# Listing the busiest expert's first four slots inside the states' layer

## The chip, the cores and the metric

The kernel runs on one core of a Trainium2 chip. The metric is the device time of one execution in microseconds (us); lower is better. The engines are TensorE (PE in the profile, with its weight loads as PEld), VectorE (DVE), ScalarE (ACT), GpSimd (POOL) and SyncE (SP), which here only issues DMAs.

## The reference, cut to what matters

Three stages stand one after another. First an attention of 8 x 8 heads, 512 rows of x and 32 states each, in both directions; it gives 8 x (512 + 32) = 4352 rows of 512 numbers. Then a gated layer, then experts:

```
x   = concat(xread, sread)            # 8 batches x 544 rows, 512 wide
x   = ((x @ w_a) * (x @ w_b)) @ w_out # 512 -> 1536 -> 512
idx = argmax(x @ w_gate, axis=1)      # one of 8 experts for each row
for e in range(8):                    # w1[e]: 512 x 1024, w2[e]: 1024 x 512
    out[idx == e] = gate * (relu(x[idx == e] @ w1[e]) @ w2[e])
```

On these inputs the reference sends 1082, 32, 576, 64, 512, 1024, 512 and 550 rows to experts 0 to 7. Of the 4096 rows that come from x (the first 512 of each batch), expert 0 gets 1024 and expert 5 gets 1024; no other has more than 512.

## The kernel before, in words

**The gated layers.** Batches 0 to 7 go through attention and the gated layer with 512 columns each. A ninth pass, b = B, is the states' layer: the 256 state rows of all batches together. Each pass has 12 steps f. In a step TensorE makes a column block of x @ w_a into AB (`first_layer`, L1279), one of x @ w_b into BB, and adds the product of the step before to YB (`second_layer`, L1292). Between them stand fills of the bank pair FB, whose order is written out by hand in tables (`TURNS`, `HEADS`, ...): in the states' layer these turn the last batch's result ("yt") and make its logits ("lg"), four of each, in steps 0 to 3. VectorE forms the product in BB (L950) and its low half gl (L958); ScalarE copies AB (L711) and the high half gh (L719). TensorE needs gl of step f for its BB matmuls of step f + 1. All matrices are split in a rounded high part and a low part, so each product takes three matmuls.

**The routing.** After each step of the states' layer VectorE runs a piece of `route_early(f)`: the 32 tiles of 128 x-rows (T1 = 32 of T = 34 tiles) are ranked within their experts, from step 3 to step 11. TensorE counts with a triangular matrix in step 5 (L1346). After the layer come the two tiles of state rows: result to SBUF (L671), transposes (L1355), logits (L1363), counts (L1371), and a chain of small VectorE instructions (L1099 to L1158), in which every one waits for the one before. It gives each row a slot (one of SLOTS = 41 tiles of 128 rows, each of one expert) and a place in it. `match` and `carry` (L1121, L1129) and a GpSimd product (L562) make the table `what`; 34 matmuls `pick` x `what` (L1379) turn it into lists: `itab` (which rows of y to gather, where to scatter), `gates`, `etab` (the expert of a slot) and `ends` (the last slot of each expert).

**The experts' loop.** Slot j takes: GpSimd copies a column of `itab` to `cur` (L542), gathers 128 rows of y from DRAM into xg (L549), TensorE turns them (`turn_x`, L1392), `up` makes HB (24 matmuls, L1406), ScalarE applies relu (L771), `turn_h` turns it (L1428), `down` makes OB (24 matmuls, L1419), ScalarE scales (`result`, L782), GpSimd scatters (L555). TensorE's order in the loop is up(j), turn_x(j+1), down(j-1), turn_h(j). xg, xgh, hth and o_sb have one buffer each.

**The weights.** SP loads an expert's 8 MB in 16 chunks of 512 KB, in the order of the experts, into one of the two halves of WS (L474); at most two chunks are in flight, since chunk n waits for chunk n - 2. The first half of the chunks serves `up`, the second `down`. Expert 0 waits for the end of the last BB matmuls, and SP stores the last result rows before it (L344). From the third expert on, its load waits until the expert two before it has gone through its last `up` (first chunk) and `down` (ninth chunk):

```
end = eng.value_load(ends[0:1, e - 2:e - 1], min_val=0, max_val=SLOTS)
if e >= 2 and c == 0:
    eng.wait_ge(s["h_mm"], end * HALVES + 1)
if e >= 2 and c == CHUNKS // 2:
    eng.wait_ge(s["o_mm"], end + 1)
```

GpSimd's loop scatters the slot that lies LAG = 4 behind the one it gathers, right after the gather is issued, and ScalarE's result(j) waits for the scatter of slot j - 1.

Of the kernel before, what the change touches and what calls it, by code (L numbers as in the profile page):

```python
# [4 lines left out]
F32 = mybir.dt.float32  # L5
# [10 lines left out]
def attention_gated_experts(nc, x, state, w_a, w_b, w_out, w_gate, w1, w2, out):  # L16
# [29 lines left out]
    EARLY = 24  # L46
    LAG = 4
    MIDDLE = TOK // 2
# [21 lines left out]
    with ctx:  # L70
# [6 lines left out]
        def sem(name):  # L77
# [23 lines left out]
        closing = ExitStack()  # L101
        turned_end = sb("turned_end", [P, DM], F32, closing)
        closing.close()
# [7 lines left out]
        stage.close()  # L111
        wraw = sb("wraw", [P, 4, 512], F32, first)
# [25 lines left out]
        pick = sb("pick", [P, EARLY, P], F32R, early)  # L138
        e3 = {n: sb(n, [P, T, E], F32, early) for n in ("lt0", "lt1", "lt2")}
        one = sb("one", [P, T, E], BF16, early)  # L140
        tot = sb("tot", [P, E, T], F32, early)
        upto = sb("upto", [P, E, T], F32, early)
        tri = sb("tri", [P, 2, P], BF16, early)
        steps = sb("steps", [P, P], F32, early)
        rev = sb("rev", [P, E], F32, early)
        zeros = sb("zeros", [P, E * T], F32, early)
        tok = sb("tok", [P, T], F32, early)
        pt = sb("pt", [P, 8, T], F32, early)
        pe8 = sb("pe8", [P, 8, E], F32, early)
        pti = sb("pti", [P, 3, T], I32, early)  # L150
# [10 lines left out]
        listing = ExitStack()  # L161
        what = sb("what", [P, T, 3 * LIST], F32R, listing)
        late = sb("late", [P, T - EARLY, P], F32R, listing)
        same = sb("same", [P, T, LIST], F32, listing)
        gate2 = sb("gate2", [P, 2, T], F32R, listing)
        cmp41 = sb("cmp41", [P, SLOTS, E], F32, listing)
        f41 = sb("f41", [P, 5, SLOTS], F32, listing)
        itab = sb("itab", [P, SLOTS + LAG, 2], I32, listing)
        ends = sb("ends", [P, E], I32, listing)
        etab = sb("etab", [P, SLOTS], I32, listing)  # L170
        cur = sb("cur", [P, 2], I32, listing)
        gates = sb("gates", [P, SLOTS], F32, listing)
        listing.close()

        xg = sb("xg", [P, DM], F32, second)
        xgh, xgl = (sb(n, [P, KC, P], F32R, second) for n in ("xgh", "xgl"))
        h_sb = sb("h_sb", [P, FE], F32, second)
        hth, htl = (sb(n, [P, FEC, P], F32R, second) for n in ("hth", "htl"))
        o_sb = sb("o_sb", [P, DM], F32, second)
        HB = ps("HB", [P, HALVES, 512], second)  # L180
        HT = ps("HT", [P, 2, 512], second)
# [14 lines left out]
            "gp_turned", "iota_ready", "memory_free", "same_ready", "rows_ready", "early_mm", "early_read", "route", "shifted", "route_exp", "one_ready",  # L196
            "pick_ready", "what_ready", "list_mm", "list_ready", "taken",
# [3 lines left out]
        reads_out, reads_in = sem("reads_out"), sem("reads_in")  # L201
# [15 lines left out]
                 (10, 0): ("a2t", 1), (10, 3): ("sr", 1), (11, 1): ("a1t", 0), (11, 2): ("a1t", 1)}  # L217
        BEGIN = {(0, 0): ("a2t", 0), (0, 2): ("sr", 0), (1, 0): ("a2t", 1), (1, 2): ("sr", 1)}
# [25 lines left out]
        def table_of(b):  # L244
            t = {}
            if b == 0:
                t |= {k: (*v, 0) for k, v in BEGIN.items()}
            else:
                t |= {k: (*v, b - 1) for k, v in TURNS.items()}
# [129 lines left out]
        def _(eng):  # L379
# [44 lines left out]
            for b in range(NB):  # L424
                for f in range(FC):
                    if f == 0 and b % 2 and b < B - 1:
                        load_state(b // 2 + 1)
                    if f == 0 and b < B - 1:
                        load_x(eng, b + 1, 0)
# [12 lines left out]
            store_y(eng, B, 0)  # L442
            store_y(eng, B, 1)

            for e in range(E):
                for i in range(DEEP):
                    eng.wait_ge(piece_out[i], 16 * pieces_before(PIECES * (e + 1), i))
                if e == 0:  # L450
                    eng.wait_ge(s["b_done"], FC * NB)
                if e == 1:
                    eng.wait_ge(s["y_mm"], FC * NB)
                if e == 2:
                    eng.wait_ge(s["list_ready"], 1)
                if e >= 2:
                    end = eng.value_load(ends[0:1, e - 2:e - 1], min_val=0, max_val=SLOTS)
                for c in range(CHUNKS):
                    if e >= 2 and c == 0:
                        eng.wait_ge(s["h_mm"], end * HALVES + 1)  # L460
                    if e >= 2 and c == CHUNKS // 2:
                        eng.wait_ge(s["o_mm"], end + 1)
                    n = CHUNKS * e + c
                    if n >= 2:
                        eng.wait_ge(chunk_in[c % 2], 16 * (n // 2))
                    part, k = c // (CHUNKS // 4), c % (CHUNKS // 4)
                    dst = WS[:, e % 2, part * PART + k * CHUNK:part * PART + k * CHUNK + CHUNK].bitcast(F32)
                    if part == 0:
                        src = w1[e, k * P:k * P + P, :]
                    elif part == 2:  # L470
                        src, dst = w2_v[e, :, 2 * k:2 * k + 2, :], dst.rearrange("p (f d) -> p f d", f=2)
                    else:
                        src = lows[e, :, part // 2, k * CHUNK:k * CHUNK + CHUNK]
# [4 lines left out]
        def _(eng):  # L478
# [53 lines left out]
            eng.wait_ge(s["y_mm"], FC * NB)  # L532
            eng.wait_ge(s["y_evac"], T)
            for i in range(2):
                eng.wait_ge(y_stored[i], 16 * (B * TS // 2) + 16 * (P // N))
            for i in range(DEEP):
                eng.wait_ge(piece_out[i], 16 * pieces_before(PIECES * E, i))
            eng.memset(itab[:, :, :], 0).then_inc(s["memory_free"], 1)

            def take(k, n):  # L540

                eng.tensor_copy(cur[:, :], itab[:, bass.ds(k, 1), :].rearrange("p a b -> p (a b)"))\  # L542
                   .then_inc(s["taken"], 1)
                if whole(n):
                    eng.wait_ge(s["memory_free"], 1)
                eng.wait_ge(s["taken"], n)
# [5 lines left out]

            def scatter():

                eng.indirect_dma_start(out=out, out_offset=bass.IndirectOffsetOnAxis(ap=cur[:, 1:2], axis=0),  # L555
                                       in_=o_sb[:, :], in_offset=None, bounds_check=TOK - 1, oob_is_err=False)\
# [8 lines left out]

            eng.wait_ge(s["list_ready"], 1)
            for k in range(LAG):
                if k:
                    eng.wait_ge(s["turn_x"], k)
                take(k, k + 1)  # L570
                gather()
                eng.wait_ge(s["gathered"], 16 * k + 16)
            eng.wait_ge(s["list_ready"], 3)
            with eng.Fori(LAG + 1, SLOTS + 1) as n:
                eng.wait_ge(s["turn_x"], n - 1)
                eng.wait_ge(s["o_ready"], n - LAG)
                take(n - 1, n)
                gather()
                scatter()
                eng.wait_ge(s["gathered"], n * 16)  # L580
                eng.wait_ge(s["scattered"], n * 16 - 16 * LAG)
            for k in range(SLOTS, SLOTS + LAG):
                eng.wait_ge(s["o_ready"], k - LAG + 1)
                take(k, k + 1)
# [893 lines left out]
```

## Time and profile before

| | us |
|---|---|
| median of 3 runs (lowest, highest) | 1397.8 (1395.91, 1399.06) |
| the profiled execution | 1394.39 |
| its span, first to last instruction | 1392.7 |
| TensorE busy | 1323.2 (95%) |
| VectorE, ScalarE, GpSimd busy | 601.9, 509.1, 357.9 |
| states' layer, from its first AB matmul to its last YB matmul | 767.3 to 824.3 |
| first `up` matmul | 858.8 |

The span is that of one profiled execution; the 1.7 us between it and the execution's own time lie around the first and the last instruction. A busy TensorE is not one at its peak: the granted clock tells at which speed it ran. The chain that ended last says which engine's work set the end at each moment; idle time of the others costs nothing.

### The profile page before, as it was taken

What the parts mean: (1) busy time and instruction counts of PE and PEld (TensorE: products, weight loads), DVE (VectorE), ACT (ScalarE), POOL (GpSimd) and SP (SyncE); (2) the same over time, 40 slices, a digit from 0 to 9 for tenths busy, and PEclk for the clock granted to TensorE, in tenths of its full rate; (3) what the DMA queues carried; (4) which work ended last, traced back from release to release, by engine and by line L of the source; (5) the groups of instructions that cost most, each with busy time, mean ns of one, the idle gap of its engine ahead of it and who ended that gap; (6) DMA issues with size and microseconds to landing.
All of it is one profiled execution on the core that took longest, in us unless ns stands there. A gap on an engine that the chain in (4) does not pass through costs nothing.

```text
span 1392.7 us, 20352 instructions
## 1 busy us (share of the span) xinstructions
PE 1323.2 (95%) x6682; PEld 1099.3 (79%) x6683; DVE 601.9 (43%) x1070; ACT 509.1 (37%) x880; POOL 357.9 (26%) x350
## 2 busy tenths in 40 slices
PE   5899999999999999999999975999899999999996
PEld 3678888888888888778888974888787888888884
DVE  4775476664765755766556454111111111111110
ACT  4453354543545534546334210222122222222221
POOL 0001244443444523434233101111111111111111
PEclk9999999999999999999999986999999999999998
DMA  6231455445545554555467217713778772361100
GB/s 200 61 93 56 135 179 176 150 161 164 152 152 182 151 176 127 165 165 147 129 221 255 70 60 247 252 33 130 245 238 262 253 252 91 113 219 45 44 26 1
DMA packets 129085, 208.22 MB, mean 150 GB/s; under 512 B 47680, under 2 KB 49728, under 8 KB 129024
## 3 DMA queue, kind: packets, MB, share of 16 engines
q1 hardware_dynamic: 86336, 148.16, 33.3%
q10 hardware_dynamic: 36128, 39.59, 9.5%
q0 software_dynamic: 6560, 19.67, 4.4%
q8 instruction: 36, 0.59, 0.2%
q14 instruction: 25, 0.20, 0.0%
HBM read 155.47 MB, written 53.74 MB: 150 GB/s over the span
## 4 chain that ended last, share of the span: by engine, by line
PE 82%; DMA 8%; DVE 5%; issue 1%; SPq 1%; ACT 1%; POOL 0%; ACTq 0%; DVEq 0%; POOLq 0%
PE YB L1292 18%; PE OB L1419 14%; PE HB L1406 14%; PE BB L1279 10%; PE AB L1279 10%; DMA WS<-in_moe_w 5%; DMA WS<-expert_lows 3%; PE FB L1254 3%; DVE SW L814 2%; PE HT L1428 2%; PE FB L1205 2%; PE FB L1240 2%; PE FB L1225 2%; PE FB L1234 1%; PE XB L1392 1%
## 5 line engine op out<-in xcount | busy, mean ns | idle before, releaser
L510 POOL TENSOR_TENSOR raw<-raw,upper 128x512 f32<-128x512 f32 x128 | 167.7, 1310 | 254.7 <-DVE upper L832 254.7
L1406 PE MATMUL HB<-WS,xgh 128*128 x656 | 210.6, 403 | 8.6 <-DMA WS<-in_moe_w 6.8
L1419 PE MATMUL OB<-WS,hth 128*128 x656 | 206.5, 396 | 3.7 <-DVE htl L1168 2.8
L1168 DVE TENSOR_TENSOR htl<-HT,hth 128x1024 fp32r<-128x1024 f32 x41 | 50.2, 1225 | 301.9 <-ACT hth L775 301.9
L1292 PE MATMUL YB<-WOh,gh 128*128 128x512 f32 x408 | 165.3, 405 | 0.1
L1279 PE MATMUL AB<-ATh,SW 128*128 128x512 f32 (+1 forms) x480 | 160.5, 383 | 2.7 <-DVE ATl L906 2.7
L1279 PE MATMUL BB<-ATh,SW 128*128 128x512 f32 (+1 forms) x480 | 158.9, 380 | 2.2 <-DVE gl L958 1.5
L1292 PE MATMUL YB<-WOh,gl 128*128 128x512 f32 x408 | 159.8, 392 | 0.0
L1292 PE MATMUL YB<-WOl,gh 128*128 128x512 f32 x408 | 159.3, 390 | 0.0
L515 POOL TENSOR_TENSOR split_ring<-wr,split_ring 128x512 fp32r<-128x512 f32 x72 | 93.1, 1293 | 252.5 <-ACT split_ring L636 252.5
L1406 PEld LDWEIGHTS HB<-WS,xgh 128*128 128x128 f32 x656 | 123.0, 193 | 34.7 <-issue 9.7
L814 DVE TENSOR_TENSOR SW<-FB,SW 64x512 fp32r<-64x512 f32 x176 | 121.1, 688 | 51.4 <-ACT SW L629 47.7
L1419 PEld LDWEIGHTS OB<-WS,hth 128*128 128x128 f32 x656 | 120.3, 188 | 28.6 <-issue 5.0
L629 ACT ACTIVATE SW<-FB 64x512 fp32r<-64x512 f32 x176 | 104.2, 592 | 83.4 <-PE FB L1254 62.3
L1406 PE MATMUL HB<-WS,xgl 128*128 x328 | 130.7, 398 | 0.0
L1419 PE MATMUL OB<-WS,htl 128*128 x328 | 128.4, 391 | 0.0
L782 ACT ACTIVATE o_sb<-OB,gates 128x512 f32<-128x512 f32 x41 | 28.2, 689 | 265.9 <-DMA out_rows<-o_sb,cur 223.3
L542 POOL COPY cur<-itab 128x2 int32 (+1 forms) x45 | 8.4, 186 | 406.1 <-PE XB L1392 369.5
L950 DVE TENSOR_TENSOR BB<-gp,BB 128x512 f32<-128x512 f32 (+1 forms) x108 | 71.6, 663 | 77.9 <-PE BB L1279 77.0
L1279 PEld LDWEIGHTS AB<-ATh,SW 128*128 128x128 f32 x480 | 87.9, 188 | 19.5 <-DVE ATl L906 3.5
L1279 PEld LDWEIGHTS BB<-ATh,SW 128*128 128x128 f32 x480 | 88.0, 189 | 18.0 <-DVE gl L958 3.0
L719 ACT ACTIVATE gh<-BB 128x512 fp32r<-128x512 f32 (+1 forms) x108 | 61.8, 573 | 102.7 <-DVE BB L950 102.0
(179 smaller groups left out, 2054.2 us busy)
## 6 DMA issues: line engine op xcount, KB each, us to landing
raw<-in_moe_w SPq DMA_DIRECT2D x128, 256.0 KB, 3.1
expert_lows<-raw SPq DMA_DIRECT2D x128, 256.0 KB, 2.1
WS<-in_moe_w SPq DMA_DIRECT2D x64, 512.0 KB, 4.3
WS<-expert_lows SPq DMA_DIRECT2D x64, 512.0 KB, 4.6
wr<-in_moe_w_b ACTq DMA_DIRECT2D x52, 256.0 KB, 2.9
wr<-in_moe_w_a ACTq DMA_DIRECT2D x49, 256.0 KB, 3.1
y_rows<-y_sb ACTq DMA_DIRECT2D x32, 256.0 KB, 3.0
xq<-in_x SPq DMA_DIRECT2D x32, 128.0 KB, 3.2
```

What stands on the lines that cost most here:

```text
L510: eng.tensor_tensor(piece, piece, upper[:, :].bitcast(F32), ALU.subtract).then_inc(s["e_lo"], 1)
L515: eng.tensor_tensor(lower(a), src, rounded(a).bitcast(F32), ALU.subtract).then_inc(s["wf_lo"], 1)
L629: eng.activation(SW[r, j, side, m, :, 2 * (k // 2), :], bank[r, :].rearrange("p (f c) -> p f c", c=P), ACT.Copy).then_inc(s["sw_hi"], 1)
L719: eng.activation(gh[:, f % 2, 0:width], BB[:, 0:width], ACT.Copy)\
L814: eng.tensor_tensor(place[:, :, c + 1, :], bank[r, :].rearrange("p (f c) -> p f c", c=P), place[:, :, c, :].bitcast(F32), ALU.subtract).th ...
L950: eng.tensor_tensor(BB[:, 0:width], gp[:, 0:width], BB[:, 0:width], ALU.mult)\
L1168: eng.tensor_tensor(htl[:, :, :], HT[:, :, :].rearrange("p a (k c) -> p (a k) c", c=P), hth[:, :, :].bitcast(F32), ALU.subtract).then_inc( ...
L1254: last = eng.matmul(bank, part[:, k, :], w, start=(i == 0), stop=(i == 2))
L1279: last = eng.matmul(bank[:, 0:width], wt, act, start=(k == 0 and i == 0), stop=(k == len(terms) - 1 and i == 2))
L1292: last = eng.matmul(YB[:, tt, :], act[:, f % 2, c], wt[:, f, :], start=(f == 0 and i == 0), stop=(f == FC - 1 and i == 2))
L1406: last = eng.matmul(HB[:, i, :], act[:, k, :], w, start=(k == 0 and m == 0), stop=(k == KC - 1 and m == 2))
L1419: last = eng.matmul(OB[:, :], act[:, k, :], w, start=(k == 0 and m == 0), stop=(k == FEC - 1 and m == 2))
```

## The change

The 32 tiles of x-rows are counted earlier: the eight fills "yt" and "lg" of the last batch are packed into steps 0 to 2 (`TURNS_LAST`), and `route_early` runs from step 2. In step 5 `first_expert` picks the expert that most x-rows chose (the lowest index of equals) and writes `order`: this expert first, then the others in their order. Slots 0 to 3 (LAG = 4) then hold this expert's first 512 x-rows, whatever the state rows do. They are listed in step 9 by 32 small matmuls of 12 columns, and their gathers and matmuls no longer wait for the last ranking.

SP loads weights in the order of `order`, whose entry is read from SBUF into a register, so the DRAM address of each chunk comes from a register. The load of the first expert waits for `order_ready` and for the BB matmuls of step 3 (its first half) and step 7 (its second half), and no longer for the stores of the last rows. Those stores move to ScalarE's queue, behind the fourth gather; so that y holds something in those rows before, the states are copied there by one DMA (`spans`) when batch 7 begins.

After the layer TensorE's order is written out by hand: turn_x(0) ahead of the last `second_layer`, then up, down and turns of slots 0 to 3, and between them the transposes, logits, counts and the 34 list matmuls. VectorE's chain has the same steps as before and some 11 small ones more; `picks` makes 8 tiles in one instruction where it took one for each. In GpSimd's loop a scatter now lies BACK = 3 slots behind its gather, waits for `result` of its slot in the same turn, and the next turn's `take` waits for that scatter to land.

```diff
+        TURNS_LAST = {(0, 0): ("yt", 0), (0, 1): ("lg", 0), (0, 2): ("yt", 1), (1, 0): ("lg", 1),
+                      (1, 1): ("yt", 2), (1, 2): ("lg", 2), (1, 3): ("yt", 3), (2, 0): ("lg", 3)}
...
+                    if k == 0 and c % (CHUNKS // 2) == 0:
+                        eng.wait_ge(s["b_done"], B * FC + (4 if c == 0 else 8))
...
+                    one_of = bass.ds(e, 1)
                     if part == 0:
-                        src = w1[e, k * P:k * P + P, :]
+                        src = w1[one_of, i * P:i * P + P, :].rearrange("e p c -> (e p) c")
...
+            for k in range(LAG):
+                if k:
+                    eng.wait_ge(s["turn_x"], k)
+                take(k, k + 1 - BACK if k >= BACK else None)
+                gather()
+                eng.wait_ge(s["gathered"], 16 * k + 16)
+            eng.wait_ge(s["o_ready"], 1)
+            scatter()
             for i, (a, c) in enumerate(((0, T // 2), (T // 2, T))):
                 eng.wait_ge(s["same_ready"], i + 1)
                 eng.tensor_tensor(what[:, a:c, 0:LIST], ...)
...
+            with eng.Fori(LAG + 1 - BACK, SLOTS + 1 - BACK) as m:
+                eng.wait_ge(s["turn_x"], m + (BACK - 1))
+                eng.wait_ge(s["scattered"], m * 16 - 16)
+                take(m + (BACK - 1), m)
                 gather()
+                eng.wait_ge(s["memory_free"], 2)
+                eng.wait_ge(s["o_ready"], m)
                 scatter()
+                eng.wait_ge(s["gathered"], m * 16 + 16 * BACK)
...
+                if f == 7:
+                    picks(pick[:, 0:8, :], 0, 8)
...                    # gate, same_early, what_early: 10 small instructions
+                if f == 8:
+                    for a in range(8, T1, 8):
+                        picks(pick[:, a:a + 8, :], a, a + 8)
...
+                    if b == B and f == 9:
+                        eng.wait_ge(s["early_what"], 3)
+                        eng.wait_ge(s["early_read"], 1)
+                        for t in range(T1):
+                            if t % 8 == 0:
+                                eng.wait_ge(s["pick_ready"], t // 8 + 1)
+                            last = eng.matmul(RB[:, 0, 0:3 * LAG], pick[:, t, :], what_early[:, t, :],
+                                              start=(t == 0), stop=(t == T1 - 1))
+                        last.then_inc(s["early_list"], 1)
+                if b == B:
+                    eng.wait_ge(s["glo_ready"], FC * NB)
+                    turn_x(0)
                 second_layer(b, FC - 1, tiles)
...
+            up(0, 0, at, (0,))
             for tt in range(TN): ...          # transposes of the state tiles
+            turn_x(1)
+            up(0, 0, at, (1,))
             for tt ...                        # logits of the state tiles
+            turn_h(0)
+            up(1, 0, at, (0,))
...                                            # counts of the state tiles
+            up(1, 0, at, (1,))
+            turn_x(2)
+            down(0, 0, at)
+            turn_h(1)
+            up(2, 0, at)
+            turn_x(3)
             for t in range(T): ...            # the 34 list matmuls
+            down(1, 0, at)
+            turn_h(2)
+            up(3, 0, at)
+            turn_x(LAG)
+            down(2, 0, at)
+            turn_h(3)
```

## Rows read from the trace of the kernel before

**Rows 1.** The page: TensorE's granted clock in 40 slices of the span, tenths.
```profile
PEclk9999999999999999999999986999999999999998
```

**Rows 2.** Stretches: length, busy PE, PEld, DVE, ACT, POOL; granted clock, DMA share, GB/s.
```profile
824.30:858.70 34.40, 12.77 (x65) 11.62 (x64) 20.06 (x65) 2.50 (x5) 5.39 (x7) 0.56 0.72 223
...
845.00:849.00 4.00, 3.90 (x18) 3.70 (x17) 1.38 (x5) 0.00 (x0) 0.00 (x0) 0.50 0.76 248
...
1062.60:1067.00 4.40, 4.36 (x13) 3.42 (x14) 1.23 (x1) 1.22 (x2) 0.00 (x0) 0.64 0.81 253
```

**Rows 3.** The chain that ended last, in order of time: start, us, what.
```profile
822.66 1.67 PE YB L1292 x6
...
868.44 5.75 PE HB L1406 x24
874.19 0.44 PE XB L1392 x4
...
887.00 5.50 PE OB L1419 x24
892.50 0.87 PE HT L1428 x8
...
906.02 5.49 PE HB L1406 x24
...
983.41 8.19 PE HB L1406 x24
```

**Rows 4.** Timeline of GpSimd and TensorE around the first gather: start, us, instruction.
```profile
850.14 1.18 POOL L549 DMA_INDIRECT xg<-y_rows,cur  x1 [0.29 <-POOL cur L542]
...
855.91 1.09 PE L1392 MATMUL XB<-ident,xg 128*128 128x128 f32 x4 [6.85 <-DMA xg<-y_rows,cur]
```

**Rows 5.** Timeline of TensorE: logits of one tile; weight loads of ten list matmuls.
```profile
785.85 0.95 PE L1240 MATMUL FB<-wg,xt 128*128 128x8 f32 x8
...
846.62 2.25 PEld L1379 LDWEIGHTS RB<-what,late 128*128 128x128 f32 x10
```

**Rows 6.** VectorE's timeline: step 8 of the states' layer, and a 714-element comparison.
```profile
808.55 0.43 DVE L950 TENSOR_TENSOR BB<-gp,BB 128x256 f32<-128x256 f32 x1 [2.21 <-PE BB L1279]
809.43 0.42 DVE L958 TENSOR_TENSOR gl<-BB,gh 128x256 fp32r<-128x256 f32 x1 [0.45 <-ACT gh L719]
...
841.05 0.90 DVE L1121 TENSOR_TENSOR same<-steps,pt 128x714 f32<-128x714 f32 x1
```

**Rows 7.** The late ranking on VectorE, first, held and last instruction; GpSimd's product beside it.
```profile
831.50 0.16 DVE L1099 TENSOR_TENSOR pe<-pe,RB 128x8 f32<-128x8 f32 x1 [0.40 <-PE RB L1371]
...
837.36 1.38 DVE L1018 TENSOR_SCALAR pt<-pt 128x2 f32<-128x2 f32 x1
...
843.42 1.70 DVE L1129 TENSOR_TENSOR what<-same,gate 128x714 fp32r<-128x714 f32 x2
...
837.33 1.39 POOL L562 TENSOR_TENSOR what<-same,tok 128x714 fp32r<-128x714 f32 x1 [6.99 <-DVE same L1121]
```

**Rows 8.** SP's queue: the last rows' stores, first chunks of experts 0 and 1.
```profile
824.98 3.63 SPq L344 DMA_DIRECT2D y_rows<-y_sb  x8
828.78 5.74 SPq L474 DMA_DIRECT2D WS<-in_moe_w  x4
...
864.65 4.66 SPq L474 DMA_DIRECT2D WS<-in_moe_w  x3
```

**Rows 9.** Who TensorE waited for from 906 to 1370: us in total, times, longest.
```profile
PE HB L1406 <- DMA WS<-in_moe_w: 6.4, 2, 3.6
```

**Rows 10.** GpSimd, ScalarE and TensorE around one late scatter in the loop.
```profile
1108.48 1.00 POOL L549 DMA_INDIRECT xg<-y_rows,cur  x1 [0.75 <-POOL cur L542]
1109.79 1.01 POOL L555 DMA_INDIRECT out_rows<-o_sb,cur  x1 [0.31 <-issue]
...
1117.00 0.69 ACT L782 ACTIVATE o_sb<-OB,gates 128x512 f32<-128x512 f32 x1 [9.01 <-DMA out_rows<-o_sb,cur]
...
1120.32 0.73 PE L1419 MATMUL OB<-WS,hth 128*128 x2 [0.33 <-DMA WS<-in_moe_w]
```

More of the change, by code:

```diff
@@ L1281, in first_layer, with expert, turn_x @@
                 last.then_inc(s[done], 1)
+            def expert(j):
+                return eng.value_load(etab[0:1, bass.ds(j, 1)], min_val=0, max_val=E - 1)
+            def turn_x(j):
+                eng.wait_ge(s["gathered"], j * 16 + 16)
+                if not (isinstance(j, int) and j == 0):
+                    eng.wait_ge(s["xgl_ready"], j)
+                for k in range(KC):
+                    last = eng.transpose(XB[:, k * P:k * P + P], xg[:, k * P:k * P + P], ident[:, :])
+                last.then_inc(s["turn_x"], 1)
@@ new lines, in down @@
+            def down(j, e, at):
+                for c in chunk_in:
+                    eng.wait_ge(c, e * (8 * CHUNKS) + 8 * CHUNKS)
+                eng.wait_ge(s["htl_ready"], j + 1)
+                if not (isinstance(j, int) and j == 0):
+                    eng.wait_ge(s["o_ready"], j)
+                for k in range(FEC):
+                    for m, (act, half) in enumerate(((hth, 0), (hth, 1), (htl, 0))):
+                        w = WSf[:, bass.ds(at + ((2 + half) * PART + k * DM), DM)]
+                        last = eng.matmul(OB[:, :], act[:, k, :], w,
+                                          start=(k == 0 and m == 0), stop=(k == FEC - 1 and m == 2))
+                last.then_inc(s["o_mm"], 1)
@@ new lines, in turn_h, with slot_of @@
+            def turn_h(j):
+                eng.wait_ge(s["h_ready"], j * HALVES + HALVES)
+                if not (isinstance(j, int) and j == 0):
+                    eng.wait_ge(s["htl_ready"], j)
+                for k in range(FEC):
+                    last = eng.transpose(HT[:, k // 4, (k % 4) * P:(k % 4) * P + P], h_sb[:, k * P:k * P + P],
+                                         ident[:, :])
+                last.then_inc(s["turn_h"], 1)
+            def slot_of(e):
+                return eng.snap((e & 1) * (4 * PART))
@@ L1410, in down @@
-            def down(j, e, at):
-                for c in chunk_in:
-                    eng.wait_ge(c, e * (8 * CHUNKS) + 8 * CHUNKS)
-                eng.wait_ge(s["htl_ready"], j + 1)
-                if not (isinstance(j, int) and j == 0):
-                    eng.wait_ge(s["o_ready"], j)
-                for k in range(FEC):
-                    for m, (act, half) in enumerate(((hth, 0), (hth, 1), (htl, 0))):
-                        w = WSf[:, bass.ds(at + ((2 + half) * PART + k * DM), DM)]
-                        last = eng.matmul(OB[:, :], act[:, k, :], w,
-                                          start=(k == 0 and m == 0), stop=(k == FEC - 1 and m == 2))
-                last.then_inc(s["o_mm"], 1)
```

494 lines of the change are left out of this document (268 added, 226 removed).

## The prediction, on record before the change was run

> **What bounds the kernel now.** I read the page first: TensorE's granted clock is full nearly throughout and dips where the states' layer hands over to the experts [rows 1]. The table of stretches shows why: of the 34.4 us between the last YB matmul of the layer and the first `up`, TensorE works 12.8, at a mean clock of 0.56 [rows 2]. Then the chain that ended last, in order of time: up to 824.33 it is TensorE's layer, from 868.44 on TensorE's slots one after another [rows 3], and between the two SP's stores and the chunks of expert 0, from 824.98 on [rows 8]. So the ranking and the weights both fill the gap; removing one alone would leave the other. A slot of the steady loop is 5.49 (up) + 0.44 (turn_x) + 5.50 (down) + 0.87 (turn_h) = 12.30 us, without a pause [rows 3]. After slot 4 TensorE waits for weights only twice, 6.4 us in all [rows 9]. TensorE's order of work sets the end, so I count its timeline from the layer to the start of up(4), before and after.
>
> **Which expert comes first.** By the counts experts 0 and 5 tie with 1024 x-rows; the lowest index wins, and `order` is the order of before. Slots, loads and their collisions after slot 4 are therefore those of before, moved as a block: each later load starts from an `up` or `down` of TensorE.
>
> **Before, layer's end to up(4):** 906.02 - 824.33 = 81.7 us [rows 3].
>
> **After, the same work on TensorE, at full clock.** Four ups 22.0, three downs 16.5, four turn_h 3.5, turn_x of slots 1 to 4 1.8 [rows 3]; two groups of state transposes 0.9 (eight at 0.11, as in turn_x); 16 logit matmuls at 0.1, 1.6 [rows 5]; two counts 0.2; 34 list matmuls. These ran at a clock of 0.50 [rows 2] with a pitch of 2.25 / 10 = 0.22 us [rows 5]; at full clock I take half, so 3.7. Sum 50.2. What stands between: turn_x(1) needs a gather that starts when turn_x(0) is done. From issue at 850.14 to TensorE's start at 855.91 the first gather took 5.8, and some 0.7 goes before for the copy [rows 4]; behind turn_x(0) TensorE has the last YB group 1.7 [rows 3], half an up 2.75 and the transposes 0.9, 5.3 in all. Stall 1.2. Together 51.4.
>
> **The other engines beside it.** VectorE's late chain ran from 831.50 to 845.1, 13.6 us, of which some 2.4 went into two instructions held beside GpSimd's two products (one of them in [rows 7]). Without the holding, and with six added ranking steps of 0.2, two xl (1.4) and one hl (1.2), it is 15.0. From the counts to the list matmuls TensorE has half an up, turn_x, down, turn_h, up and turn_x: 2.75 + 0.44 + 5.5 + 0.87 + 5.5 + 0.44 = 15.5. The second half of `what` is wanted only after 17 of the list matmuls, at 17.4. So the ranking is hidden, by 2.4 us; uncovered, each us of it is a us of the sum. The tables behind it (1.3) and the fifth gather with its wait for the stores (6.5) lie under down(1), turn_h(2) and up(3), 11.9. GpSimd reaches its products after scatter 0, some 8 us behind turn_x(2), and needs 2.8 [rows 7] of a cover of 12.3. ScalarE's eight stores take 3.6 as SP's did [rows 8], while down(1) runs; queued behind them is result(1), not wanted for 5 us.
>
> **Weights.** `order` is ready after step 5, near 798.5 (step 8's low half is done at 809.85 [rows 6], three steps of 4.3 back is 797.0, then eight small instructions). 16 chunks took 864.65 - 828.78 = 35.9 [rows 8]: half by 817, all by about 836. up(0) starts near 828, down(0) near 844: hidden with 11 and 8 us to spare.
>
> **The longer layer.** 32 matmuls of 12 columns cost their weight loads, 0.10 to 0.11 at full clock [rows 5]: 3.5. turn_x(0) 0.4. "lg" 2 now waits for VectorE's copy of "yt" 2, about 0.3. In a step VectorE's product and low half are done 1.3 us after BB [rows 6], and TensorE wants the low half 2.8 after it, so 2.9 us of routing fit and 4.3 with the slack used up. Steps 2, 5 and 6 get 2.6 each, step 7 3.9 (a comparison of 1024 elements is 1.25 by the row of 714 in 0.90 [rows 6], and ten small ones), step 8 3 x 1.25 = 3.8. Steps 7 and 8 use the slack one after the other; the 0.3 too much falls under the early list. Layer +4.2; bounds 3.5 and 7.
>
> First gain: 81.7 - 51.4 - 4.2 = 26.1 us.
>
> **Corrections.** (a) Clock. After TensorE's first wait for weights an up took 8.19 in place of 5.49, 2.7 more [rows 3]; after the second the clock was 0.64 over 4.4 us, 1.6 more [rows 2]. The list matmuls of before, 7.7 us of them, never raised the clock from 0.50 [rows 2], so narrow ones seem to count for little: 32 of them in step 9 may bring it from 2.4 to 1.2 GHz, the 34 later ones less likely. 0.7 x 2.2 + 0.3 x 2.2 = -2.2; bounds 0 and -7. (b) Chunk addresses from a register: none of SP's DMAs has one here. The nearest rows are GpSimd's gathers, 0.29 behind the copy with a constant address [rows 4], 0.75 with a register [rows 10]. So 0 to 0.46 a chunk; I take 0.2. It shows where TensorE waits for weights, twice, behind 8 chunks with two in flight, 4 links each: 8 x 0.2 = -1.6; bounds 0 and -3.7. (c) In the loop result(j) waited for a scatter issued late (1109.79 to 1117.00), and through hth and htl that held TensorE until 1120.32 [rows 10]; now the scatter goes out with its result. Four such stalls of 0.1 to 0.6: +1.0; bounds 0 and 1.5. (d) After the last result a copy and 0.75 behind it [rows 10] stood ahead of the scatter; +0.6. (e) Behind a wait a group is 0.2 longer (5.75 against 5.49 [rows 3]); six such places: -1.3. The DMA of the states (512 KB, one issue) and the memsets cost nothing: the weight pieces queued behind it on SP have three buffers and no reader on TensorE; uncovered it would be the time of one chunk, 4.5.
>
> Sum: 26.1 - 2.2 - 1.6 + 1.0 + 0.6 - 1.3 = 22.6. The profiled execution took 1394.39, so 1371.8; that lies 3.4 under the median, and I keep the distance: 1375.
>
> **A rule against the change.** An instruction of VectorE on two elements took 1.38 and ended with GpSimd's product of 1.39 [rows 7]. The Trainium skill (SBUF — State Buffer, Who interferes with whom) says that the two engines share a pair of ports under an exclusive lock, and that the one that comes later is blocked for the other's whole instruction; the trace agrees. By it the two products, which now fall beside `carry`, hold VectorE for up to 2.8, 0.4 more than the cover: 22.2; without it 22.6.
>
> **Rivals.** *Forecast:* 1370 to 1380, chance 0.60. *Held and slowed* (0.12): scatter 0 is late too, so that the whole 2.8 of GpSimd's products shows, and the clock falls at both lists (2 x 2.7 in place of 2.2): 22.6 - 2.8 - 3.2 = 16.6, 1381. For it the thin cover; against it that groups of 0.8 us of logit matmuls leave the clock. *The weight stream becomes the bound* (0.12): at 1 us more per chunk both waits grow by 4 and the fourth expert after by some 4: 12 less, 1387. Against: 0.46 is the largest such row. *The ring, the other side* (0.07): a loop turn now waits for its predecessor's scatter. From the end of down(j-2) a result and issue (1.1), a scatter to landing (7.2 [rows 10]), copy and gather (1.4 and 5.8 [rows 4]) come before turn_x(j): 15.5 us, where TensorE has 18.7 of its own. Above 15.5 + 3.2 each slot pays, and with 0.6 a slot (22.6 / 37) the gain is gone: the two landings decide, slower from 16.8 together (13.0 now). At 17.0 it is 0.8 a slot, 30 in all: 1405. Against: 41 slots show no such spread. *It doesn't do what it says* (0.04): the early list or the first gather is late by steps, up(0) starts 10 to 20 us later: 1385 to 1397. *Better* (0.05): no clock fall, no address cost, 26 or more: 1369 to 1371.
>
> **The numbers.** The likeliest case gives 1375. The range takes in "better", "held and slowed" and the lower half of the weights' rival: 1369 to 1386. Within 0.2% (2.8 us, about what a measurement here can tell) ends only the far end of the fifth rival: 0.03. Slower 0.08: the ring, and a little for what I have not seen. Faster 0.89.
>
> **What would show it.** Right: first chunk issued near 799; last YB group of the layer near 826 to 828, turn_x(0) just ahead of it; up(4) near 880; a dip of the clock between 817 and 822; two waits for weights as before. Wrong: TensorE idle over 2 us at the 34 list matmuls (ranking), at turn_x in the loop (ring), over 6 us at up(10) (addresses), or BB matmuls waiting for gl in steps 8 to 10.

## The result

The changed kernel takes 1376.45 us (median of 4 runs, 1375.29 to 1378.15), the kernel before in the same session 1397.13 (4 runs, 1395.91 to 1399.06): a ratio of 0.9852, 95% interval 0.9835 to 0.9869. The forecast was 1375, range 1369 to 1386. A later session with the same kernel unchanged (below) gave 1372.45 against 1394.86, 0.9826 (0.9799 to 0.9852).

### The profile after

The page of the changed kernel, its span and the clock of TensorE in 40 slices, beside [rows 1]:

```profile
span 1373.6 us, 20473 instructions
...
PE 1328.7 (97%) x6714; PEld 1102.4 (80%) x6715; DVE 607.7 (44%) x1078; ACT 513.9 (37%) x880; POOL 358.0 (26%) x350
...
PEclk9899999999999999999999999999999999999998
```

The dip at the hand-over, two slices at 8 and 6 in [rows 1], is gone. There is a new 8 in the second slice, long before the change; I come back to it. The chain that ended last, in order of time (start, us, what), from the start of the states' layer:

```profile
766.80 5.44 PE YB L1431 x24
772.24 1.43 PE AB L1367 x12
...
818.05 1.39 PE YB L1431 x6
819.44 3.47 PE RB L1494 x32
822.91 2.23 PE AB L1367 x12
825.15 2.23 PE BB L1367 x12
827.38 1.39 PE YB L1431 x6
...
834.86 5.35 DMA xg<-y_rows,cur
...
840.25 0.66 PE XB L1379 x4
840.90 2.79 PE HB L1393 x12
...
858.85 5.59 PE HB L1393 x24
864.44 0.44 PE XB L1379 x4
864.87 3.74 PE RB L1542 x34
868.62 5.53 PE OB L1406 x24
...
874.93 6.28 DMA xg<-y_rows,cur
881.26 0.66 PE XB L1379 x4
...
888.26 5.59 PE HB L1393 x24
```

This is to be read in three places. The early list takes 3.47 us and the 24 products behind it 4.46 where such a pair takes 2.87: the clock fell. Then TensorE's slots follow at once; two transfers are still on the chain, the second and the fifth gather, and TensorE stands idle for 0.85 and 0.7 us at their ends. And up(4) starts at 888.26, against 906.02 in [rows 3].

The table of stretches of the changed kernel (length, busy PE, PEld, DVE, ACT, POOL; granted clock, DMA share, GB/s): the two groups behind the early list, the end of the layer to up(4), and the 34 list products:

```profile
822.90:827.40 4.50, 4.50 (x26) 4.50 (x26) 0.62 (x5) 0.39 (x1) 1.33 (x2) 0.62 0.82 229
835.20:888.26 53.06, 51.28 (x277) 43.07 (x278) 24.88 (x66) 13.77 (x22) 10.77 (x13) 1.00 0.75 236
864.80:868.60 3.80, 3.80 (x36) 3.80 (x35) 3.45 (x10) 0.76 (x2) 0.00 (x0) 1.00 0.85 226
```

Where [rows 2] had TensorE busy 12.8 of 34.4 us at a clock of 0.56, it is now busy 51.3 of 53.1 at 1.00.

**The account.** I split both profiled executions at the start of the layer (end of the 24 YB products: 767.43 before, 772.24 after) and at up(4).

| stretch | before | after | difference |
|---|---|---|---|
| start to layer | 767.43 | 772.24 | +4.8 |
| the layer, to its last YB | 56.9 | 62.9 | +6.0 |
| last YB to up(4) | 81.7 | 53.1 | -28.6 |
| up(4) to the end | 486.6 | 485.3 | -1.3 |
| span | 1392.65 | 1373.56 | -19.1 |

From the layer to up(4) it is 138.6 against 116.0. The first line is not the change's. A group of 32 products at the very start, the same work in both kernels, took longer in the second profile, and by the first YB group of twelve behind it all of the 4.8 us is there (chain of before, then of the changed kernel):

```profile
14.84 4.15 PE FB L1205 x32
...
60.46 2.76 PE YB L1292 x12
...
767.43 1.43 PE AB L1279 x12
```

```profile
14.92 6.91 PE FB L1293 x32
...
65.21 2.76 PE YB L1431 x12
```

This group sorts all fourteen profiles of this study. It takes 3.7 to 4.3 us in seven (before, e5, e7 to e11 below), whose layer starts between 767.4 and 770.3, and 6.8 to 6.9 in the other seven (the changed kernel, c1, e1 to e4, e6), whose layer starts between 771.5 and 773.4. Versions of both kernels stand in both groups. The mean clock of the first 60 us, 0.97 in the profile of before and 0.91 in that of after, does not sort them: it is 0.97 in e6 too, whose layer starts last of all. The cause of the two starts is not shown. Since the span of one execution carries some 4 us of it, I compare the experiments by the part from the layer's start to the end as well: 625.2 before, 601.3 after.

### The profile page after: what moved, and what is told of

Same layout as the page of the kernel before. It is cut to its first block, busy times and chain, and to the rows that moved or that the text cites. A ratio compares the mean times of both kernels' runs of the same rounds, so it can differ in the third digit from the quotient of the medians.

```text
span 1373.6 us, 20473 instructions
## 1 busy us (share of the span) xinstructions
PE 1328.7 (97%) x6714; PEld 1102.4 (80%) x6715; DVE 607.7 (44%) x1078; ACT 513.9 (37%) x880; POOL 358.0 (26%) x350
## 3 DMA queue, kind: packets, MB, share of 16 engines
q1 hardware_dynamic: 85968, 148.16, 34.2%
## 4 chain that ended last, share of the span: by engine, by line
PE 88%; DVE 5%; DMA 3%; issue 1%; ACT 1%; SPq 1%; POOL 0%; ACTq 0%; DVEq 0%; POOLq 0%
PE YB L1431 18%; PE HB L1393 16%; PE OB L1406 16%; PE BB L1367 10%; PE AB L1367 10%; PE FB L1342 3%; PE HT L1415 2%; PE FB L1293 2%; DVE SW L856 2%; PE FB L1328 2%; PE FB L1313 2%; PE XB L1379 1%; PE FB L1322 1%; PE FB L1285 1%; PE FB L1338 1%
## 5 line engine op out<-in xcount | busy, mean ns | idle before, releaser
L721 ACT ACTIVATE h_sb<-HB 128x512 f32<-128x512 f32 x82 | 49.0, 597 | 168.3 <-PE HB L1393 168.3
L1164 DVE TENSOR_TENSOR xgl<-XB,xgh 128x512 fp32r<-128x512 f32 x41 | 28.3, 691 | 177.5 <-ACT xgh L713 177.4
```

The source lines that it names most:

```text
L721: eng.activation(h_sb[:, i * 512:i * 512 + 512], HB[:, i, :], ACT.Relu).then_inc(s["h_ready"], 1)
```

## The experiments

Twelve runs. "Layer to end" is the span less the start of the layer, from the profiled execution.

| run | median us | ratio to before (95%) | layer to end |
|---|---|---|---|
| before | 1394.6 to 1398.8 | | 625.2 |
| c1 changed kernel again | 1372.45 | 0.9826 (0.9799 to 0.9852) | 601.0 |
| e1 weights late | 1389.96 | 0.9956 (0.9932 to 0.9980) | 618.4 |
| e2 weights early | 1395.94 | 1.0000 (0.9985 to 1.0015) | 625.1 |
| e3 HT first | 1394.51 | 1.0005 (0.9983 to 1.0026) | 621.0 |
| e4 xgh moved | 1401.80 | 1.0017 (0.9995 to 1.0039) | 629.8 |
| e5 list split | 1371.29 | 0.9807 (0.9778 to 0.9836) | 598.2 |
| e6 stores sooner | 1375.87 | 0.9823 (0.9795 to 0.9851) | 601.7 |
| e7 fixed order | 1372.74 | 0.9801 (0.9776 to 0.9826) | 601.1 |
| e8 xgh 128 bytes on | 1399.63 | 1.0012 (0.9988 to 1.0036) | 626.6 |
| e9 rows aligned | 1370.88 | 0.9806 (0.9774 to 0.9839) | 597.7 |
| e10 list, stores, rows | 1370.07 | 0.9808 (0.9774 to 0.9842) | 594.9 |
| e11 all at 192 | 1372.40 | 0.9855 (0.9818 to 0.9892) | 598.3 |

The versions of the kernel before scatter over some 5 us in the last column once the 3.3 us of e4's and e8's moved rows (below) are taken off, because a wait for weights that ends a microsecond later can take the clock with it. The profile of before is itself a lucky one by 1.6 us: behind the last wait for `htl`, 2.8 us in every profile, the last `down` takes 7.17 to 7.40 us in thirteen of the fourteen profiles and 5.76 in this one alone. The changed kernel's two profiles lie closer (601.3 and 601.0).

### The changed kernel again (c1)

> The changed kernel once more, nothing altered. Two things are asked of it. The time: 0.985 of the kernel before, 1375 to 1378 us. The start: in the profile of the changed kernel the states' layer began at 772.24, in that of the kernel before at 767.14, and in the first 25 us the granted clock was 0.5 for 10.24 us against 3.4 us. If that is chance of the clock's phase in one execution, this profile shows another length of the stretch at 0.5 and the layer begins near 767; if the change itself does it (another program at the start), it begins at 772 again.

Measured 1372.45 us, below the expected 1375 to 1378; the ratio, 0.9826, is near the 0.985. The layer starts at 772.23 again, and the fall behind the early list is there again, so that fall is no accident. By this profile alone the late start would be put down to the change; the experiments on the kernel before (e2 to e4: 771.55, 771.48, 772.02) and those on the changed one that start early (e5, e7, e9 to e11: 768.7 to 770.3) show that it isn't. The profile of before, 767.43, had the earliest start of all fourteen.

### The list without the weights (e1)

```diff
                     if k == 0 and c % (CHUNKS // 2) == 0:
-                        eng.wait_ge(s["b_done"], B * FC + (4 if c == 0 else 8))
+                        eng.wait_ge(s["b_done"], FC * NB)
```

> The listing half of the change alone: the first expert's sixteen chunks wait for the whole layer again, as in the kernel before. By the forecast's account the weights are then the path: the list is ready at 819 and the gather lands near 850, but the first chunk is issued at about 835 and the last of sixteen 36.5 us later, and up(0) begins some 30 us behind the first issue, near 865 instead of 835. Expected 17 to 19 us slower than the changed kernel (1393 to 1396 us, a gain of 1 to 5 us against before). The rival, that the gain comes from the list alone and the weights have slack in the stream, expects no more than 3 us of loss (1376 to 1380 us).

1389.96 us, 17.5 above the changed kernel's 1372.45; from the layer to the end 618.4 against 601.0, 17.4 more: the 17 to 19 expected. The time itself missed the expected 1393 to 1396 us, which were reckoned from 1376 and not from 1372. SP issues the first chunk at 831.35, where the changed kernel did it at 805.16. The waits of TensorE from 835 on:

```profile
PE HB L1393 <- DMA WS<-expert_lows: 17.9, 2, 16.6
```

One wait of 16.6 us ahead of up(0). The clock falls in it: the first half of up(0) takes 5.48 us for 12 products. The rival, that the weights had slack, is out. The list alone is worth 6.8 us of layer to end, 4.9 by the medians of its session (1394.86 against 1389.96).

### The weights without the list (e2)

```diff
                 for c in range(CHUNKS):
+                    if e == 0 and c % (CHUNKS // 2) == 0:
+                        eng.wait_ge(s["b_done"], B * FC + (4 if c == 0 else 8))
```

Beside it the wait for the whole layer is gone, and the last rows' stores stand ahead of expert 1's chunks.

> The weights half of the change alone: the kernel before, with its first expert's chunks issued after the layer's first step group and the last rows' stores moved behind them. By the forecast's account the first up is bound there by ranking, list and gather in a row (PE free at 822.7, up at 850 to 868), so that earlier weights free nothing at once, and only the 12.0 us of later waits for weights shrink: 1 to 3 us faster than before, 1394 to 1396 us. The rival, that the weights were a part of the bound before, expects over 6 us faster, under 1391 us.

1395.94 us, ratio 1.0000; layer to end 625.1. My 1 to 3 us did not come. (The 12.0 us of later waits in it are too much: the waits for weights are 8.9 us from 835 on, 6.7 of them behind slot 4.) The first chunk goes out at 790.22 and the sixteenth by 822.3, but TensorE still waits 9.8 us for `what` and 6.8 us for the first gather:

```profile
PE RB L1379 <- DVE what L1129: 9.8, 1, 9.8
PE XB L1392 <- DMA xg<-y_rows,cur: 6.8, 1, 6.8
```

The weights alone give 0.1, the list alone 6.8, both together 24; by the medians of that session -1.1, 4.9 and 22.4. A profile of before with the common last `down` would add 1.6 to each of the three figures from profiles. Behind either limit lay the other, as the forecast said.

### Where up's 5.58 us comes from (e3, e4, e8, e9, e11)

In the changed kernel every whole `up` takes 5.58 to 5.60 us at full clock (5.59 above), against 5.49 in [rows 3], in the same 24 products; `down` (5.50) and the turns are as before. At 0.09 us for 37 slots that is 3.3 us which no step of my forecast has. Two things about its operands had changed that the forecast didn't look at: which banks of PSUM hold `HB`, and where xgh and xgl lie in SBUF.

**e3**, the banks, in the kernel before:

```diff
-        HB = ps("HB", [P, HALVES, 512], second)
         HT = ps("HT", [P, 2, 512], second)
+        HB = ps("HB", [P, HALVES, 512], second)
```

> The kernel before with one thing altered: in PSUM the tile HT stands before HB, as it does in the changed kernel, so that the up products accumulate in other banks. In the changed kernel a half of up takes 5.58 us in place of 5.49, in all 37 slots (0.09 us x 37 = 3.3 us). If the banks do it, this kernel shows 5.58 too and is 3.3 us slower than before (1400 us). If it is the place in SBUF of the gathered rows, or anything else, it shows 5.49 and the time of before (1396 to 1398 us).

All but the groups behind a wait stay at 5.49; ratio 1.0005. Not the banks. (Its 621.0 from layer to end goes with shorter waits for weights behind slot 4, 3.4 us where the profile of before has 6.7 counted in the same way, and with one fall of the clock behind them in place of two; at the last `down` it has the fall that the profile of before lacks.)

**e4**, the place, in the kernel before:

```diff
+        rows = ExitStack()
+        sb("until_xgh", [P, DM], F32, rows)
+        xgh, xgl = (sb(n, [P, KC, P], F32R, rows) for n in ("xgh", "xgl"))
+        rows.close()
         wraw = sb("wraw", [P, 4, 512], F32, first)
...
-        xgh, xgl = (sb(n, [P, KC, P], F32R, second) for n in ("xgh", "xgl"))
+        sb("in_place_of_xgh", [P, 2 * DM], F32, second)
```

> The kernel before with one thing altered: xgh and xgl, the split rows that up multiplies, lie in SBUF where the changed kernel has them (behind the normalisation's buffers, 38 KB further up a partition); everything else stays where it was. The run with the banks exchanged kept a half pair of up at 5.49 us, so of the two suspects the place in SBUF is left. If it is the cause, up takes 5.58 us here and the 37 slots cost 3.3 us more than before (ratio 1.002). If it is not (something else of the changed kernel's program), up stays at 5.49 and the time is that of before.

Now the kernel before has it; the chain of e4:

```profile
923.61 5.58 PE HB L1410 x24
...
929.63 5.50 PE OB L1423 x24
```

So it is the place. The time is 1401.80, ratio 1.0017, of the expected size, but its interval (0.9995 to 1.0039) holds 1: the durations show it, not the time. Adding up the allocations gives the byte within a partition: xgh at 134720 in the kernel before, 173760 in the changed one, WS at 1600 in both. Modulo 256 that is 64, 192 and 64.

**e8**, in the kernel before, 128 bytes and no other region:

```diff
+        sb("until_xgh", [P, 32], F32, second)
         xgh, xgl = (sb(n, [P, KC, P], F32R, second) for n in ("xgh", "xgl"))
+        sb("until_h", [P, 480], F32, second)
```

> The kernel before with xgh and xgl 128 bytes further up each partition (and nothing else moved against 2048 bytes). With the two where the changed kernel has them, all the up products of the kernel before went from 5.49 to 5.58 us. Two things differ between the places: the region (134720 against 173760 bytes) and the offset within 256 bytes (64 against 192; the weights WS, hth and htl lie at 64). If the offset does it, up takes 5.58 us here, 37 x 0.09 = 3.3 us more than before. If the region does it, up stays at 5.49.

The chain of e8:

```profile
1115.54 5.58 PE HB L1408 x24
```

128 bytes are enough, and the region is not needed. The time, ratio 1.0012, is of the expected sign, but its interval holds 1, and layer to end is 1.4 more and not 3.3, within the scatter of these profiles.

**e9**, the changed kernel, with its rows at 64 again:

```diff
-        wg = sb("wg", [P, KC, E], F32, first)
         stage = ExitStack()
...
         wraw = sb("wraw", [P, 4, 512], F32, first)
+        wg = sb("wg", [P, KC, E], F32, first)
```

> The changed kernel with the 128 bytes of wg allocated behind wraw in place of ahead of it, so that xg, xgh and xgl lie 128 bytes lower in each partition, in the same region, at offset 64 within 256 bytes as WS does. If the offset makes up slower, up is back at 5.49 us and the kernel is 3.3 us faster than the changed one from the states' layer to the end (601.0 to 601.4 there, so 598; ratio to before 0.980). If the region does it, up stays at 5.58 and nothing changes.

The chain of e9:

```profile
1101.83 5.49 PE HB L1393 x24
...
1107.76 5.50 PE OB L1406 x24
```

Layer to end 597.7, 3.3 and 3.6 less than the two profiles of the changed kernel: the 3.3 us expected. Two accidents about cancel in it: its gathers were late by 0.2 us, not 1.5 and 2.1, and the clock fell at both waits for weights, so that one up more took 7.3. The median of whole runs, 1370.88, can't tell 3 us from the spread of the start.

**e11** asks whether it is one operand's offset or the two operands' difference:

```diff
         logits = sb("logits", [P, T, E], F32)
+        wg = sb("wg", [P, KC, E], F32)
...
-        wg = sb("wg", [P, KC, E], F32, first)
```

> The changed kernel with the 128 bytes of wg allocated at the very front, so that every large tensor that PE reads (SW, WOh, gh, WS, xgh, hth) lies at offset 192 within 256 bytes, in place of 64 for all but xg, xgh and xgl. It asks what the 5.58 us of up came from. If what counts is that the two operands of a product lie at different offsets (xgh at 192, WS at 64), up is back at 5.49 us, down stays at 5.50, and the layer to the end takes 598 us as with the rows at 64. If what counts is the offset of an operand by itself, the products that stay at 1.36 us for six in every run so far go to 1.39 as well, down to 5.58, and the kernel is some 2% slower than the changed one (1395 to 1405).

The chain of e11:

```profile
1101.08 5.47 PE HB L1393 x24
...
1106.99 5.50 PE OB L1406 x24
```

With xgh and WS both at 192 `up` takes 5.47, the fastest of all, and nothing else is slower. So xgh at 192 is not slow by itself: 64 with 64 and 192 with 192 run at 5.49 and 5.47, 192 with 64 at 5.58. Layer to end 598.3, though two gathers were late by 2.8 us here. The other mix (xgh at 64, WS at 192) and other differences than 128 bytes weren't tried, so that any difference costs is not shown, and no run shows the mechanism behind it.

### The early list in two halves (e5)

```diff
+                    if b == B and f == 9:
+                        list_early(0, T1 // 2)       # between step 9's AB and BB
...
-                        for t in range(T1):          # all 32 behind step 9's YB
+                        list_early(T1 // 2, T1)
```

> The changed kernel with the early list's 32 narrow products in two halves: sixteen between the two first-layer products of step 9 and sixteen where all 32 stood. Both profiles of the changed kernel show the granted clock at 0.5 for one stretch of 3.41 us right behind these 32 products, and 24 products of the next step take 4.46 us in place of 2.86. If the row of narrow work brings the clock down, the stretch is gone and the kernel is 1.6 us faster than the changed one (1370.5 to 1371.5, ratio to before about 0.981). The rival, that the number of narrow products counts and not their place, or that the clock falls there anyway: the stretch stays and the time is that of the changed kernel, 1372.5.

The chain of e5 (from the second half of the layer's step 9), and its stretches from there:

```profile
816.36 1.54 PE BB L1367 x12
817.90 1.39 PE YB L1442 x6
819.29 1.69 PE RB L1429 x16
820.98 1.53 PE AB L1367 x12
822.50 1.44 PE BB L1367 x12
```

```profile
819.29:826.76 7.47, 7.47 (x61) 7.21 (x60) 1.50 (x8) 0.77 (x2) 1.33 (x2) 1.00 0.75 245
```

The clock stays at 1.00; the pair behind the list takes 2.97 where it took 4.46 and a pair elsewhere 2.87. 1371.29 us, in the expected range. Layer to end 598.2, 2.8 to 3.1 less, more than the 1.6 expected; the rest is that no gather was late in this execution, where the changed kernel lost 1.5 and 2.1 to them. The clock fell for 32 narrow products in a row and not for twice sixteen.

### ScalarE's stores sooner (e6)

```diff
+            eng.wait_ge(s["gathered"], 16 * LAG)
+            for tt in range(TN):
+                store_y(eng, B, tt)
             for j in range(2, LAG):
                 relu(j)
                 xh(j + 1)
-                if j == 2:
-                    ...
```

> The changed kernel with ScalarE's eight stores of the last rows ahead of slot 2's relu in place of behind it, 3.8 us of issue moved some 10 us earlier. In the changed kernel the fifth gather is held until they have passed, and its turn waits 0.8 us (2.1 us in the second profile). Expected: that wait gone, 0.5 to 2 us faster than the changed kernel. The rival: the issue now holds slot 2's relu, the up behind it waits, and it is 1 to 3 us slower.

601.7 from layer to end, 1375.87 us: nothing gained. The expectation had misread one profile: the fifth gather held TensorE 0.7 us in the first profile of the changed kernel and not at all in c1, whose 2.1 us lie at the second gather. Here the fifth gather is not late either. But the second gather was, by 1.5 us (TensorE's timeline of e6, in brackets what it waited for):

```profile
842.12 0.66 PE L1378 MATMUL XB<-ident,xg 128*128 128x128 f32 x4 [1.53 <-DMA xg<-y_rows,cur]
```

This wait was 0.85 in the first profile of the changed kernel; it moves with how long that gather takes. Inconclusive between 0 and 0.8 us; the rival's loss of 1 to 3 us is not seen.

### Addresses by constants (e7)

```diff
-                e = eng.value_load(order[0:1, k:k + 1], min_val=0, max_val=E - 1)
...
-                    one_of = bass.ds(e, 1)
+                    one_of = slice(k, k + 1)
```

> The changed kernel with the weights' chunks addressed by constants, expert 0 first, in place of a register loaded from the order (where the two orders differ, a slot multiplies with another expert's weights; the number of products and of bytes is the same). The changed kernel issues 16 chunks in 36.5 us against 35.9 before. If the register addresses are paid once a chunk on a stream that PE waits for, the stream is 0.6 us shorter an expert and the waits for weights behind slot 4 (4.5 us) shrink by up to 3: 0 to 3 us faster than the changed kernel. If the landings set the pace and not the issues, nothing changes (within 0.5 us).

The price stands in the chain, where one chunk's landing lets the next be issued. The chain of the changed kernel at the third expert, then of e7 (start, us, what):

```profile
944.09 4.64 DMA WS<-in_moe_w
...
948.74 0.04 SPq L490
...
948.82 0.03 SPq L490
...
948.88 4.39 DMA WS<-in_moe_w
```

```profile
941.68 4.78 DMA WS<-in_moe_w
...
946.48 4.48 DMA WS<-in_moe_w
```

From a landing to the next transfer it is 0.15 us with a register address, with two small steps of SP between them, and 0.02 with a constant: 0.13 a chunk. The time of sixteen chunks doesn't show it. The first expert's took 36.5 in the changed kernel and 34.2 in e7, but it is 34.8 to 37.1 in the eight profiles with register addresses and 34.2 to 35.9 in the five with constants whose stream nothing else holds. TensorE's waits for weights behind slot 4 are 4.2 us in e7 against 4.5 and 3.8, and layer to end is 601.1: no wait shows the price. (In this data the order is that of the constants, as the forecast worked out, so each slot multiplies with the same expert in both.)

### All three (e10)

The diffs of e5, e6 and e9 together.

> The changed kernel with the early list split in two halves, ScalarE's stores ahead of slot 2's relu, and the rows at offset 64. The split list gave 2.8 us from the states' layer to the end (598.2 against 601.0 and 601.4); the stores alone gave nothing that the time shows (601.7); the offset is to give 3.3 us. If the three add up, the layer to the end takes 595 us and the time is 1366 to 1369 (ratio to before about 0.978). The rival: the faster slots run into the weights, whose waits of 4 us then grow by as much as the offset gives, and it stays at 598 (ratio 0.980).

594.9 from layer to end, as expected, 6.1 and 6.4 less than the changed kernel; the waits for weights stay at 4.3, so the stream doesn't take it back. The median of 6 runs is 1370.07, a microsecond above the range of 1366 to 1369 and 28.7 below the 1398.78 of before in that session (ratio 0.9808). That is the fastest version, but against c1's ratio of 0.9826 the intervals overlap: only the profiles show the 6 us, the times do not prove them.

## Why the prediction was right, step by step

**What bounds it: right.** Both limits filled the gap; e1 and e2 show it with 6.8 and 0.1 against 24 (medians: 4.9 and -1.1 against 22.4).

**The sum to up(4): right, 51.4 forecast and 53.1 measured.** The 34 products at full clock took 3.74 (3.7 forecast), the stall at turn_x(1) 0.85 (1.2). About 0.9 of the difference I had under (e), whose six places of 0.26 make 1.6 and not 1.3. Missing were a second stall of 0.7 at turn_x(4) and the slower ups (0.09 each). The fifth gather's cover, 11.9 for 7.8, was thinner than I counted: GpSimd's copy waited until 873.98 for the last of the eight stores to land ("9.93 <-DMA y_rows<-y_sb" in its timeline).

**The layer: +4.2 and 2.2 for the clock forecast, +6.0 measured.** The early list took 3.47 (3.5), the clock behind it 1.6 and not 2.2; the rest is turn_x(0) and "lg" 2. The fall that I gave a chance of 0.7 came in all seven profiles where the 32 products stand together; at the 34 products, 0.3, the clock did not fall. That the 2.2, a mean over two falls of which one came, lies near the 1.6 is partly luck.

**The late ranking: right, but barely.** VectorE's chain started at 849.20 and the list products at 864.87 without a pause. GpSimd's two products held VectorE as forecast. VectorE's and GpSimd's timelines:

```profile
849.20 0.16 DVE L1190 TENSOR_TENSOR pe<-pe,RB 128x8 f32<-128x8 f32 x1 [0.58 <-PE RB L1528]
...
861.43 4.20 DVE L1223 TENSOR_TENSOR what<-same,gate 128x714 fp32r<-128x714 f32 x2
```

```profile
861.28 2.77 POOL L592 TENSOR_TENSOR what<-same,tok 128x714 fp32r<-128x714 f32 x2
```

Two such products took 1.70 in [rows 7] and 1.71 here at 858.67 (in the same timeline); beside GpSimd's 2.77 they take 4.20, 2.5 more. The Trainium skill (SBUF — State Buffer, Who interferes with whom) says that the pair of ports the two engines share is an exclusive lock; this row agrees. The 0.4 it would have cost didn't show, for the chain was shorter than reckoned: 16.4 us from 849.20 to 865.63 with the holding in it, where the forecast has 15.0 + 2.8. The second half of `what` was wanted after 17 of the list products, at 866.7: 1.1 us to spare.

**The weights: right.** The first chunk went out 32.9 us after the layer's start, where 31.1 was forecast, and up(0) did not wait for it.

**After up(4): the terms were mis-sized, their sum nearly right.** Forecast -1.6 (b), +1.0 (c), +0.6 (d), -0.4 (two of the six places of (e)): -0.4. Measured +1.3. (b) The address is paid, 0.13 a chunk and not 0.2, but no wait grew by it: 4.5 us of waits behind 880 against 6.4 in [rows 9]. And behind the first of them the clock did not fall, so the two ups behind the waits took 5.84 and 7.39. Before they took 8.19 and 7.3 (the 1.6 that (a) reads from the stretch at 0.64 is 1.9 over the whole up). Against 5.58 and 5.49 that is 2.1 and 4.6: 2.5 better. This is the luck of an execution and no work of the change: e9, with the same order of loads, had both falls. (c) is there, and larger than forecast. In the profile of before the four slots with a late scatter, from the up at 1101.13 to that at 1151.99, took 50.9 us where four of 12.30 are 49.2: 1.7, not 1.0. None of this is left in the changed kernel, where ScalarE's `result` waits for no scatter. GpSimd's timeline shows the loop, a scatter at once with its result:

```profile
1063.08 0.99 POOL L569 DMA_INDIRECT xg<-y_rows,cur  x1 [0.76 <-POOL cur L562]
1069.06 1.01 POOL L577 DMA_INDIRECT out_rows<-o_sb,cur  x1 [4.99 <-ACT o_sb L732]
1075.03 0.18 POOL L562 COPY cur<-itab 128x2 int32 x1 [4.95 <-DMA out_rows<-o_sb,cur]
```

(d) From the last OB product to the end of the span it is 10.7 against 11.1: 0.3 in place of 0.6. Against these stand two things that I didn't have: up's 3.3 us, and the last `down`, 7.39 at a fallen clock where the profile of before had 5.76 (chain of before, then of after):

```profile
1375.81 5.76 PE OB L1419 x24
```

```profile
1355.43 7.39 PE OB L1406 x24
```

The second is no effect of the change: every other version of the kernel before has the fall there too. In sum 1.9 + 2.5 + 1.7 + 0.3 - 3.3 - 1.6 = 1.5 for the 1.3 measured.

**The rivals.** The ring did not close: the take at 1075.03 waits for the scatter, but the turn that needs its gather is at 1086.04, and TensorE waits for no gather behind slot 4. The weights' stream and "held and slowed" did not come either: the clock fell at one list of two.

**The time itself.** Against its own profile the forecast was 1371.8 and the profiled execution took 1375.29. From the layer on, the forecast gain of 22.6 stands against 23.9 in the two profiles, 1.3 better; the start, 4.8 worse, makes up the 3.5 us. By the medians the gain is 20.7 in the first session and 22.4 in c1's. The step that was missing altogether is the operands' new place. It cost 3.3 us of 24, and was offset by shorter waits for weights, one fall of the clock fewer and the larger (c): the mechanism was right, but that the sum comes so near is in part luck.

## What to carry to other kernels

When two limits fill one gap, cost the change by what both removals give together, and expect little of either alone: 6.8 and 0.1 us, but 24 in one. When a change moves an operand of the matmul that repeats most, look at its byte offset against its partner's as part of the change, and compare the duration of one group before and after; here it is worth 3.3 us for a moved line. Before reading a difference of a few microseconds from two profiles, split both at a point ahead of the change: here 4.8 us of the difference lay before it.

## What the runs showed of the hardware

The offset: 24 fp32r products of 128x128 by 512 columns took 5.49 us with both operands at byte 64 of 256 and 5.47 with both at 192, but 5.58 with the stationary one at 192 and the moving one at 64. The clock: 32 products of 12 columns in a row (3.47 us) were followed by a fall from 2.4 to 1.2 GHz in each of the seven profiles where they stand together, twice sixteen with 2.9 us of wide products between them by none (e5, e10), and the 34 products of 126 columns (3.74 us) of the changed kernel by none. With the DRAM address of SP's DMAs in a register, 0.15 us lay between one chunk's landing and the next transfer, with a constant 0.02.
